# Reading of the states with x as the stationary operand and the weights divided ahead of their turn, in a float32 pipeline on one core

## The reference

```python
scores2 = scale * np.matmul(state, x.transpose(0, 1, 3, 2))   # 32 x 512 per head
scores2 = scores2 - scores2.max(-1, keepdims=True)
a2 = np.exp(scores2)
a2 /= a2.sum(-1, keepdims=True) + 1e-09
sread = np.matmul(a2, x)                                        # 32 x 64 per head
```

## Time and profile before

| | |
|---|---|
| median of 3 runs | 1248.16 us |
| the profiled execution | 1246.85 us |
| its span in the trace | 1245.1 us |
| TensorE (matmul) busy | 1237.0 us, 99% |
| VectorE, ScalarE busy | 800.1 us (64%), 548.5 us (44%) |
| loads and stores | 63.76 MB, 51 GB/s over the span |

### The profile page before, as it was taken

One profiled execution on the slowest core, in us unless ns is written; L12 is line 12 of the kernel. 1 busy time (PEld: TensorE's weight loads), 2 busy tenths in 40 slices (PEclk: granted clock), 3 DMA queues, 4 the chain that ended last, 5 costly groups with the idle time before them and its releaser, 6 DMA issues.

```text
span 1245.1 us, 17116 instructions
## 1 busy us (share of the span) xinstructions
PE 1237.0 (99%) x6636; PEld 1004.5 (81%) x6636; DVE 800.1 (64%) x1295; ACT 548.5 (44%) x1028; POOL 1.3 (0%) x7
## 2 busy tenths in 40 slices
PE   9999999999999999999999999999999999999998
PEld 7779777777777778888888888888888888888887
DVE  4656556555555445878676676676676776766776
ACT  6663434333333334555444444444444444444444
POOL 0000000000000000000000000000000000000000
PEclk9999999999999999999999999999999999999999
DMA  9941000000000111311101001001001001010000
GB/s 354 372 172 52 35 34 1 34 35 1 34 35 1 68 71 49 93 60 34 51 18 40 12 18 52 1 18 51 0 17 51 8 8 51 17 42 0 9 34 18
DMA packets 17630, 63.76 MB, mean 51 GB/s; under 512 B 1968, under 2 KB 3376, under 8 KB 12960
## 3 DMA queue, kind: packets, MB, share of 16 engines
q1 hardware_dynamic: 16832, 62.00, 13.6%
q10 hardware_dynamic: 704, 0.85, 0.2%
q0 software_dynamic: 32, 0.07, 0.0%
HBM read 45.09 MB, written 17.83 MB: 51 GB/s over the span
## 4 chain that ended last, share of the span: by engine, by line
issue 100%; POOLq 0%; POOL 0%
POOLq L261 0%; POOL ident L434 0%; POOL ident L432 0%; POOLq L434 0%; POOLq L1469 0%
## 5 line engine op out<-in xcount | busy, mean ns | idle before, releaser
L1256 ACT ACTIVATE hq<-bank 128x512 f32<-128x512 f32 (+1 forms) x144 | 82.8, 575 | 393.8 <-PE bank L1382 393.8
L1327 DVE TENSOR_TENSOR hw<-hw,hq 128x512 f32<-128x512 f32 (+1 forms) x144 | 95.5, 663 | 193.5 <-ACT hw L1267 193.4
L1382 PE MATMUL bank<-ysp_hi,wi_hi 128*128 128x512 f32 (+1 forms) x576 | 217.4, 377 | 0.0
L1382 PE MATMUL bank<-ysp_lo,wi_hi 128*128 128x512 f32 (+1 forms) x576 | 217.2, 377 | 0.0
L1382 PE MATMUL bank<-ysp_hi,wi_lo 128*128 128x512 f32 (+1 forms) x576 | 217.2, 377 | 0.0
L1409 PE MATMUL wide<-wz_hi,gsp_hi 128*128 128x512 f32 x544 | 212.3, 390 | 0.3 <-DVE gsp_lo L1317 0.3
L1409 PE MATMUL wide<-wz_lo,gsp_hi 128*128 128x512 f32 x544 | 211.8, 389 | 0.0
L1409 PE MATMUL wide<-wz_hi,gsp_lo 128*128 128x512 f32 x544 | 211.7, 389 | 0.0
L1382 PEld LDWEIGHTS bank<-ysp_hi,wi_hi 128*128 128x128 f32 x576 | 108.2, 188 | 21.3 <-DVE gb L1346 0.9
L1382 PEld LDWEIGHTS bank<-ysp_lo,wi_hi 128*128 128x128 f32 x576 | 108.3, 188 | 20.6
L1382 PEld LDWEIGHTS bank<-ysp_hi,wi_lo 128*128 128x128 f32 x576 | 108.3, 188 | 19.9
(11 more groups left out here) (122 smaller groups left out, 1740.7 us busy)
## 6 DMA issues: line engine op xcount, KB each, us to landing
xT<-in_x_cols SPq DMA_DIRECT2D x8, 1024.0 KB, 10.2
xs<-in_x_rows SPq DMA_DIRECT2D x8, 1024.0 KB, 9.6
y_dram<-ysb SPq DMA_DIRECT2D x8, 1024.0 KB, 3.9
out<-ysb SPq DMA_DIRECT2D x8, 1024.0 KB, 4.6
yr<-y_dram SPq DMA_DIRECT2D x28, 256.0 KB, 4.0
w_raw<-in_moe_w SPq DMA_DIRECT2D x8, 512.0 KB, 11.2
wi_raw<-in_moe_w_in SPq DMA_DIRECT2D x4, 1024.0 KB, 6.5
raw<-in_moe_w_out SPq DMA_DIRECT2D x16, 256.0 KB, 2.6
```

The costliest lines, as they stand in the source:

```text
L1256: act.activation(hq[:, f % 2, 0:w], ph[f % 2][:, 0:w], ACT.Square).then_inc(sq_done, 1)
L1327: dve.tensor_tensor(u, u, q, ALU.mult).then_inc(w2_done, 1)
L1382: mm = pe.matmul(ph[f % 2][:, 0:w], wi[s][c][:, f * P:(f + 1) * P], ysp[k][u][c][:, 0:w], start=c + m == 0, stop=c == KC - 1 and m == LAST)
```

## The change

The reading is computed with x as the stationary operand (128 x 64) and the turned weights as the moving one (128 x 32), into two column tiles of the array. Its result comes out as features by states, which is the form that `srs` wants. So `sread_turn` and `copy_sr` go, with the tile `sr`; ScalarE and VectorE split the result straight from the PSUM, where the batches alternate between two places (`reading(e)`). The division by the sum moves ahead of the turn: VectorE multiplies the exponentials by the inverse sums (`scale_a2`, two instructions of 128x512 per batch), `tokens_invert` moves behind `tokens_max` of its own batch, and `a2_turn` waits for the scaled weights. The order of SyncE's loads is another one, and the identity is turned 28 times at the start instead of 36.

```diff
-WARM = 36
+WARM = 28
...
+    def reading(e):
+        return ps[:, e % 2 * W:e % 2 * W + P].rearrange("p (q n) -> p q n", n=NS)
...
     def sync(sp):
...
         load_w3(sp, 1)
-        load_xT(sp, 0)
+        for e in range(2):
+            load_xT(sp, e)
         load_w3(sp, 2)
-        load_xT(sp, 1)
         load_xs(sp, 0)
         load_sT(sp, 2)
         load_xT(sp, 2)
         load_w3(sp, 3)
         load_xs(sp, 1)
         load_xT(sp, 3)
+        for n in (0, 1):
+            load_w(sp, n)
         load_w3(sp, 4)
-        load_w(sp, 0)
-        for e in range(2, 5):
-            load_xs(sp, e)
-            load_xT(sp, e + 2)
-            load_w(sp, e - 1)
-            if e < 4:
-                load_w3(sp, e + 3)
+        load_xs(sp, 2)
+        load_xT(sp, 4)
+        for n in (2, 3):
+            load_w(sp, n)
+        load_w3(sp, 5)
+        load_xs(sp, 3)
+        load_xT(sp, 5)
+        load_w(sp, 4)
+        load_w3(sp, 6)
+        load_xs(sp, 4)
+        load_xT(sp, 6)
+        load_w(sp, 5)
         load_xs(sp, 5)
+        load_w3(sp, 7)
         load_xT(sp, 7)
-        load_w3(sp, 7)
-        for n in (4, 5):
-            load_w(sp, n)
-        load_xs(sp, 6)
         for n in (6, 7):
             load_w(sp, n)
-        load_xs(sp, 7)
+        for e in (6, 7):
+            load_xs(sp, e)
...
-        def copy_sr(e):
+        def split_sr(e):
             act.wait_ge(sread_done, e + 1)
-            act.wait_ge(tok_inv, e + 1)
-            after(act, sr_turned, e)
-            for g in range(G):
-                act.activation(sr[:, g * D:(g + 1) * D], ps[:, g * D:(g + 1) * D], ACT.Copy, scale=tinv[:, g:g + 1]).then_inc(sr_copied, 1)
-
-        def split_sr(e):
-            act.wait_ge(sr_turned, e + 1)
...
+            act.activation(srs[0][:, :, e * NS:(e + 1) * NS], reading(e), ACT.Copy).then_inc(sr_hi, 1)
...
             if e >= 2:
-                copy_sr(e - 2)
+                split_sr(e - 2)
             copy_st(e)
-            if e >= 3:
-                split_sr(e - 3)
...
-        copy_sr(B - 2)
-        split_sr(B - 3)
+        split_sr(B - 2)
         turn_a2(B - 1)
         empty_prod(B - 1)
-        split_sr(B - 2)
-        copy_sr(B - 1)
         split_sr(B - 1)
...
+        def scale_a2(e):
+            dve.wait_ge(tok_inv, e + 1)
+            for g in range(G):
+                dve.tensor_scalar(a2[:, g, :], a2[:, g, :], tinv[:, g:g + 1], None, ALU.mult).then_inc(a2_scaled, 1)
...
+        tokens_invert(0)
+        scale_a2(0)
         for e in range(1, B):
...
-            tokens_invert(e - 1)
+            if e >= 2:
+                split_sr(e - 2)
             tokens_max(e)
...
+            tokens_invert(e)
+            scale_a2(e)
+            if e == 1:
+                split_w3(3)
+            if e == 6:
                 split_w3(7)
...
         def a2_turn(e):
-            pe.wait_ge(tok_exp, 2 * e + 2)
+            pe.wait_ge(a2_scaled, 2 * e + 2)
...
-            after(pe, sr_copied, 2 * e)
-            for g in range(G):
+            after(pe, sr_lo, e - 1)
+            for q in range(Q):
                 for j in range(J):
-                    for q in range(Q):
+                    for g in range(G):
                         at = q * P + g * D
-                        mm = pe.matmul(ps[q * NS:(q + 1) * NS, g * D:(g + 1) * D], a2T[:, g, j, q * NS:(q + 1) * NS],
-                                       xsb[e % 2][:, j, at:at + D], start=j == 0, stop=j == J - 1)
+                        mm = pe.matmul(reading(e)[g * D:(g + 1) * D, q, :], xsb[e % 2][:, j, at:at + D],
+                                       a2T[:, g, j, q * NS:(q + 1) * NS], start=j == 0, stop=j == J - 1)
             mm.then_inc(sread_done, 1)
-
-        def sread_turn(e):
-            pe.wait_ge(sr_copied, 2 * e + 2)
-
-            after(pe, sr_lo, e)
-            pe.transpose(ps[:, W:W + P], sr[:, :], ident[:, :]).then_inc(sr_turned, 1)
```

More of the change, by code:

```diff
@@ L302, in stage_front @@
     ident = small("ident", [P, P])
-    sr = small("sr", [P, P])
     tmax = small("tmax", [P, G])
@@ L361, in stage_front @@
     a2_turned, a2T_out = sem("a2_turned"), sem("a2T_out")
-    sread_done, sr_copied, sr_turned = (sem(n) for n in ("sread_done", "sr_copied", "sr_turned"))
+    a2_scaled, sread_done = sem("a2_scaled"), sem("sread_done")
     sr_hi, sr_lo, s1_am, s1_hi = sem("sr_hi"), sem("sr_lo"), sem("s1_am"), sem("s1_hi")
@@ L489, in turn_a2 @@
                 act.activation(a2T[:, g, :, :], pt[g].rearrange("p (j c) -> p j c", c=P), ACT.Copy).then_inc(a2T_out, 1)
-        def copy_sr(e):
+        def split_sr(e):
             act.wait_ge(sread_done, e + 1)
-            act.wait_ge(tok_inv, e + 1)
-            after(act, sr_turned, e)
-            for g in range(G):
-                act.activation(sr[:, g * D:(g + 1) * D], ps[:, g * D:(g + 1) * D], ACT.Copy, scale=tinv[:, g:g + 1]).then_inc(sr_copied, 1)
-        def split_sr(e):
-            act.wait_ge(sr_turned, e + 1)
-            act.activation(srs[0][:, :, e * NS:(e + 1) * NS], ps[:, W:W + P].rearrange("p (q n) -> p q n", n=NS), ACT.Copy).then_inc(sr_hi, 1)
+            act.activation(srs[0][:, :, e * NS:(e + 1) * NS], reading(e), ACT.Copy).then_inc(sr_hi, 1)
         load_wo(act, 0)
@@ L594, in tokens_invert @@
             dve.wait_ge(tok_exp, 2 * e + 2)
-            after(dve, sr_copied, 2 * e)
+            after(dve, a2_scaled, 2 * e)
             dve.tensor_scalar(tinv[:, :], tsum[:, :], GUARD, None, ALU.add).then_inc(tok_guard, 1)
@@ L602, in split_sr @@
             at = slice(e * NS, (e + 1) * NS)
-            dve.tensor_tensor(srs[1][:, :, at], ps[:, W:W + P].rearrange("p (q n) -> p q n", n=NS), plain(srs[0][:, :, at]), ALU.subtract
+            dve.tensor_tensor(srs[1][:, :, at], reading(e), plain(srs[0][:, :, at]), ALU.subtract
                               ).then_inc(sr_lo, 1)
@@ L644, in vector @@
         split_w(1)
-        tokens_invert(B - 1)
-        split_sr(B - 3)
+        split_sr(B - 2)
         empty_prod(B - 1)
-        split_sr(B - 2)
         split_sr(B - 1)
@@ L765, in tensor @@
             scores(e + 1)
-            if e >= 2:
-                sread_turn(e - 2)
             a2_turn(e)
@@ L770, in tensor @@
         sread(B - 2)
-        sread_turn(B - 3)
         a2_turn(B - 1)
         pieces(4 * NF1 - 1, 4 * NF1)
-        sread_turn(B - 2)
         sread(B - 1)
         values.tensor_unit(pe, 0, 0, pv)
-        sread_turn(B - 1)
         pe.wait_ge(prod_lo, NF1)
```

## The result

The changed kernel takes 1252.07 us (median of 7 runs, 1251.48 to 1253.19) against 1247.95 us for the kernel before in 7 runs: a ratio of 1.0037, 95% interval 1.0027 to 1.0047, or 4.1 us slower. The forecast was 1252.0 us. Its profiled execution took 1252.51 us, with a span of 1250.7 us.

The account below looks back on a forecast made before the run. TensorE was taken as the bound, with a matmul in flight for 1237.0 of 1245.1 us. The terms -1.5 - 2.1 + 0.5 + 6.9 gave +3.8 us, 1252.0 us, range 1244.9 to 1254.9.

Parts of the forecast that it names:

- The reading decides, by its weight load: Front, eight readings: loading 64 columns sets a step of 0.055 us, 1.89 us a reading, 6.9 us more in all.
- the two load rates: Weight loads in the rows: 0.81 ns per column in L724, 0.32 in the identity's turns; the slow one taken for the reading.
- The turns of the reading: Front, TensorE: 0.17 us six times, then 0.23 and 0.26 us, all go; 1.5 us less.
- The waits: Front, TensorE: waits of 1.4 us for `srs_lo`, 0.4 for w3 and 0.3 for xT go; 2.1 us less.
- The start: Batches 0 and 1: w3 block 2 lands 0.5 us later behind xT; the first turn of a2 starts 0.5 us later.
- The scaling: VectorE, two instructions per batch, 421 ns each (other end 610): batch 0's turn 0.5 us later, covered in later batches.
- 28 turns, worth nothing: Kernel start: eight fewer identity turns end 0.86 us earlier, but pieces still wait for w_out until 9.35 us; no gain.
- Hidden loads: Rival, chance 0.24: in the reading, 64 columns load within the 27 ns of moving; reading 1.06 us, total -2.85 us, 1245.3.

## Why the prediction was right

- *The reading decides, by its weight load.* Right, and shown from both sides. The step was put at 0.055 us and is 0.059 (load 138 ns, expected 137); a reading at 1.89 us and is 1.99. So the term of 6.9 us is 8 x 0.96 = 7.7: 0.8 too small. The row that broke the tie between the two load rates was the longer first matmul of a burst, 24 ns for 32 columns in the earlier trace rows. The working was a little loose: its rates of 0.75 and 0.81 ns per column make 48 to 52 ns for 64 columns, and the 0.055 us stood above both. The Trainium skill (TensorE: Matmul & The Clock Gate, LDWEIGHTS) gives 53 ns for 64 columns; the step measured here is 6 ns above that.
- *The turns of the reading*, 1.5 us: gone, as counted.
- *The waits*, 2.1 us: gone. For `srs_lo` the prediction named the turn's going and the order of loads, and either is enough. For w3 and xT it named the order first and longer readings beside it; with the old order they go as well. With short readings the new order takes the same three waits away and puts one of 1.2 us in their place, which I had not seen.
- *The start*: w3 block 2 is split at 18.11 instead of 17.66, the turn of a2 starts at 21.88 instead of 21.43; 0.5 was forecast. Part of such a difference is scatter, as the run with the old order shows.
- *The scaling* is 484 ns, between my ends of 421 and 610, and hidden.
- *28 turns, worth nothing*: right in the front and wrong in the whole. The prediction took the stages behind 82.47 us for untouched. The change pays 1.0 us there, which no term had, and the kernel before pays 7.8 us for the same 28 turns. Front terms measured: 7.7 - 2.1 - 1.5 + 0.45 = 4.55, of 4.58 in the trace. The span grew by 5.6 us and the medians by 4.1; the profiled execution of before lay 1.1 us under its median and that of the change 0.4 over, so the total met the forecast more closely than its terms did. That the time was met within 0.1 us is luck: the reading's 0.8 and the late 1.0 us were both missed, and scatter between executions took most of it back. That the reading gets slower by its wider load, and by how much a step, is not luck.
- *Hidden loads* was the best rival, and the swap that the Trainium skill (TensorEngine Tiling (Array Packing), Performance Considerations) advises for a narrow right side is what loses here: it halves what moves and doubles what is loaded, and the load was already half a step.

## What to carry to other kernels

For small float32 matmuls in column tiles, compare per tile and step the columns moved with the columns loaded; swapping the operands pays only while the load stays the shorter. A gain made of waits belongs to the schedule in which it was measured: try it in the other one before crediting a part of the change. And when a kernel with loops gets slower by microseconds that no edited stage shows, look at the starts of the loops' rounds for stops with no releaser, and at the number of instruction fetches in the later rounds; a handful of instructions ahead of the loop can move them.

## What was not expected of the hardware

Eight matmuls more or fewer ahead of a loop moved the whole time by 7.8 us (kernel before, 28 turns instead of 36: 1255.24 against 1247.41) and by 3.5 us the other way (changed kernel, 36 instead of 28), with the stops some 800 us later. The 7.8 us go with 58 instruction fetches instead of 40; the 3.5 us do not, since both kernels have 58, and only the stops are longer. And in a dense stretch of 128 small matmuls with their loads, run while the loads from memory fill the DMA engines, TensorE stopped for 3.4 us and then had a mean clock of 0.57 for the next 4 us.
